# An MoE routing loop: the equality products go from VectorE to GpSimd, and the room left per expert from a running PSUM sum to a tile in SBUF

## What is computed

```python
logits = x @ w_gate                      # 1536 tokens, 8 experts
order = np.argsort(-logits.flatten())
for idx in order:
    tok, e = (int(idx) // E, int(idx) % E)
    if assigned[tok] >= 0 or counts[e] >= cap:     # cap = 192
        continue
    assigned[tok] = e
    counts[e] += 1
```

## Time and profile before

| | us |
|---|---|
| median of three runs | 922.08 |
| the three runs | 913.54, 922.09, 922.08 |
| time of the profiled execution | 913.54 |
| its span in the trace | 911.9 |
| outside the span (difference) | 1.6 |

### The profile page before, as it was taken

One profiled execution on the slowest core, in us unless ns is written; L12 is line 12 of the kernel. 1 busy time (PEld: TensorE's weight loads), 2 busy tenths in 40 slices (PEclk: granted clock), 3 DMA queues, 4 the chain that ended last, 5 costly groups with the idle time before them and its releaser, 6 DMA issues.

```text
span 911.9 us, 16773 instructions
## 1 busy us (share of the span) xinstructions
PE 751.2 (82%) x5353; PEld 661.4 (73%) x5354; DVE 381.5 (42%) x913; ACT 280.4 (31%) x536; POOL 99.1 (11%) x114
## 2 busy tenths in 40 slices
PE   3999996444444099999999667999999999999993
PEld 2898995334443099999999565887788788888882
DVE  5444443999988000000000382644444462536221
ACT  2455653000000022332222302443344452535210
POOL 2000000000000500000000001222122212122220
PEclk9999997555555589999999857999999999999997
DMA  9700002900000446666660301645264453454211
GB/s 219 206 2 1 1 2 70 407 35 0 0 0 0 163 138 212 230 228 224 244 231 27 110 0 36 214 128 149 57 202 136 138 160 93 127 138 120 53 27 30
DMA packets 63908, 103.91 MB, mean 114 GB/s; under 512 B 22336, under 2 KB 24384, under 8 KB 63872
## 3 DMA queue, kind: packets, MB, share of 16 engines
q1 hardware_dynamic: 54896, 80.05, 26.9%
q0 software_dynamic: 8976, 23.39, 10.0%
HBM read 87.64 MB, written 16.57 MB: 114 GB/s over the span
## 4 chain that ended last, share of the span: by engine, by line
PE 73%; issue 18%; DMA 3%; DVE 2%; POOL 1%; ACT 0%; SPq 0%; DVEq 0%; POOLq 0%; ACTq 0%
PE PS L737 12%; PE PS L739 11%; PE PS L738 11%; PE PS L670 9%; PE PS L659 8%; PE PS L502 4%; PE PS L465 3%; PE PS L482 3%; PE PS L733 3%; DMA XE<-routed_rows 2%; PE PS L717 2%; PE PS L726 1%; PE PS L443 1%; POOL routed_rows L391 1%; PE PS L680 1%
## 5 line engine op out<-in xcount | busy, mean ns | idle before, releaser
L1141 DVE TENSOR_TENSOR WS<-STAGE,WS 128x1024 f32 (+1 forms) x64 | 74.7, 1221 | 232.6 <-ACT WS L872 197.1
L737 PE MATMUL PS<-WS,XH 128*128 128x512 f32 x216 | 89.7, 415 | 3.9 <-DVE XL L1257 2.0
L620 PE MATMUL PS<-OH,arena 128*128 128x8 bf16 x1008 | 39.8, 169 | 61.2 <-DVE arena L1119 59.2
L659 PE MATMUL PS<-XTm,arena 128*128 128x192 f32 x512 | 88.4, 333 | 1.1 <-ACT XTm L855 1.1
L737 PE MATMUL PS<-WS,HH 128*128 128x512 f32 x216 | 88.8, 411 | 0.0
L659 PEld LDWEIGHTS PS<-XTm,arena 128*128 128x128 f32 x512 | 85.8, 195 | 1.3 <-issue 1.3
L739 PE MATMUL PS<-WS,XL 128*128 128x512 f32 x216 | 85.4, 395 | 0.0
L670 PE MATMUL PS<-HTm,arena 128*128 128x192 f32 x512 | 84.8, 327 | 0.5 <-ACT HTm L861 0.5
L738 PE MATMUL PS<-WS,XH 128*128 128x512 f32 x216 | 85.0, 394 | 0.0
L739 PE MATMUL PS<-WS,HL 128*128 128x512 f32 x216 | 84.6, 392 | 0.0
L738 PE MATMUL PS<-WS,HH 128*128 128x512 f32 x216 | 84.4, 391 | 0.0
(11 more groups left out here) (227 smaller groups left out, 1140.7 us busy)
## 6 DMA issues: line engine op xcount, KB each, us to landing
arena<-in_moe_w SPq DMA_DIRECT2D x16, 2048.0 KB, 8.9
STAGE<-in_moe_w SPq DMA_DIRECT2D x128, 256.0 KB, 4.8
XE<-routed_rows SPq DMA_DIRECT2D x8, 390.8 KB, 9.8
arena<-in_v SPq DMA_DIRECT2D x12, 256.0 KB, 6.4
out<-YO POOLq DMA_DIRECT2D x1, 3072.0 KB, 20.3
first_mixture<-YR POOLq DMA_DIRECT2D x16, 192.0 KB, 4.4
arena<-in_q SPq DMA_DIRECT2D x2, 1024.0 KB, 7.7
arena<-in_k SPq DMA_DIRECT2D x2, 1024.0 KB, 8.5
```

The costliest lines, as they stand in the source:

```text
L620: ins = pe.matmul(PS[:, 6, u * E:(u + 1) * E], CMP[:, t, u * P:(u + 1) * P], OH[:, t, :], start=False, stop=(t == NT - 1 and u == NT - 1), ...
L659: ins = pe.matmul(PS[:, 2 + f % 2, 0:CAP], W1[:, pp, c, f * P:(f + 1) * P], XTm[:, c, :], start=(c == 0), stop=(c == KD - 1))
L737: pe.matmul(acc, high, w_high, start=first, stop=False)
L1141: dve.tensor_tensor(part(1), STAGE[:, slot].rearrange("p o w f -> p (o w) f"), part(0).bitcast(F32), ALU.subtract)\
```

## The change

`TOTB` goes, `NEW` and `ROOM` come. `ROOM` holds for each expert the places that are left, begins at 192 and is kept in SBUF in fp32; PE no longer carries sums from one round to the next. The equality step leaves DVE: POOL gets a loop of its own over the 7 rounds, which waits for all three parts of `VROW`, makes `EQ` in 12 instructions of 128 columns, waits for them, and makes `EQD` in one of 1536. `PER` goes from 11 to 16.

```diff
         ASG = sb("ASG", [P, NT, E], BF16)
         UNA = sb("UNA", [P, NT])
-        TOTB = sb("TOTB", [P, E], BF16)
+        NEW = sb("NEW", [P, NT])
+        ROOM = sb("ROOM", [P, E])
         RED = sb("RED", [P, E])
         PEN = sb("PEN", [P, E])
...
                            YO[:, 0:1, :].broadcast_to([P, NT, DM])).then_inc(sm["yscat"], 16)
 
-            pool.memset(TOTB[:], 0.0).then_inc(sm["totb"], 1)
+            with pool.Fori(0, E - 1) as ph:
+                pool.wait_ge(sm["vrow"], ph * 3 + 3)
+                pool.sem_inc(sm["pool_held"], 1)
+                for t in range(NT):
+                    ins = pool.tensor_scalar(EQ[:, t * P:(t + 1) * P], VROW[:, t * P:(t + 1) * P], V[:, t:t + 1], None,
+                                             ALU.is_equal)
+                ins.then_inc(sm["pool_seq"], 1)
+                pool.wait_ge(sm["pool_seq"], ph + 1)
+                pool.tensor_tensor(EQD.rearrange("p (t n) -> p t n", t=NT), EQ.rearrange("p (t n) -> p t n", t=NT),
+                                   mid(upto[:], NT), ALU.mult).then_inc(sm["eqd"], 1)
 
             pool.wait_ge(sm["slot"], 1)
...
                               start=False, stop=False, skip_group_check=True)
 
-            pe.wait_ge(sm["totb"], 1)
-            pe.matmul(PS[:, 7, 0:E], ones_b[:], TOTB[:], start=True, stop=False, skip_group_check=True).then_inc(sm["tot"], 1)
             with pe.Fori(0, E - 1) as ph:
 
...
                                            V[:, 4 * c + i:4 * c + i + 1].broadcast_to([P, P]), ident[:])
                     ins.then_inc(sm["vr_done"], 1)
-                pe.wait_ge(sm["totb"], ph + 2)
-                pe.matmul(PS[:, 6, 0:NT * E], ones_b[:], mid(TOTB[:], NT), start=True, stop=False, skip_group_check=True)
                 for t in range(NT):
                     if t == NT - 1:
...
                     for u in range(NT):
                         ins = pe.matmul(PS[:, 6, u * E:(u + 1) * E], CMP[:, t, u * P:(u + 1) * P], OH[:, t, :],
-                                  start=False, stop=(t == NT - 1 and u == NT - 1), skip_group_check=True)
+                                  start=(t == 0 and u == 0), stop=(t == NT - 1 and u == NT - 1), skip_group_check=True)
                 ins.then_inc(sm["cnt"], 1)
                 pe.wait_ge(sm["noh"], ph + 1)
-                for t in range(NT):
-                    ins = pe.matmul(PS[:, 7, 0:E], ones_b[:], NOH[:, t, :], start=False, stop=(t == NT - 1), skip_group_check=True)
-                ins.then_inc(sm["tot"], 1)
+                pe.matmul(PS[:, 7, 0:NT * E], ones_b[:], NOH[:].rearrange("p t e -> p (t e)"), start=True, stop=True)\
+                    .then_inc(sm["tot"], 1)
 
             pe.wait_ge(sm["dstart"], 1)
...
             dve.wait_ge(sm["const"], NCONST)
             link(dve.memset(UNA[:], 1.0))
+            link(dve.memset(ROOM[:], float(CAP)))
             link(dve.memset(ASG[:], 0.0))
             link(dve.tensor_copy(LM[:], L0[:]))
             start = count[0]
-            PER = 11
+            PER = 16
             with dve.Fori(0, E - 1) as ph:
                 done = [0]
...
                 linked(dve.tensor_reduce(V[:], LM[:], AX.X, ALU.max))
                 dve.sem_inc(sm["best"], 1)
-                dve.wait_ge(sm["tot"], ph + 1)
-                dve.tensor_scalar(TOTB[:], bank(7, E), 1.0 / P, None, ALU.mult).then_inc(sm["totb"], 1)
                 linked(dve.tensor_tensor(EQW[:], LM[:], bc(V[:], E), ALU.is_equal))
                 linked(dve.tensor_tensor(EQW[:], EQW[:], mid(first[:], NT), ALU.mult))
...
                         greater(t)
                 dve.wait_ge(sm["vrow"], ph * 3 + 3)
-                dve.tensor_tensor(EQ.rearrange("p (t n) -> p t n", t=NT), VROW.rearrange("p (t n) -> p t n", t=NT), bc(V[:], P),
-                                  ALU.is_equal).then_inc(sm["eq"], 1)
-                dve.wait_ge(sm["eq"], ph + 1)
-                dve.tensor_tensor(EQD.rearrange("p (t n) -> p t n", t=NT), EQ.rearrange("p (t n) -> p t n", t=NT),
-                                  mid(upto[:], NT), ALU.mult).then_inc(sm["eqd"], 1)
                 for t in range(NT):
                     n = (t + 1) * P
...
                     ins.then_inc(sm["cmp"], 1)
                 dve.wait_ge(sm["cnt"], ph + 1)
-                linked(dve.tensor_reduce(VB[:], bank(6, NT * E).rearrange("p (t e) -> p t e", t=NT), AX.X, ALU.max))
-                dve.scalar_tensor_tensor(out=NOH[:], in0=bc(VB[:], E), scalar=CAP + 0.5, in1=OH[:], op0=ALU.is_lt, op1=ALU.mult)\
-                    .then_inc(sm["noh"], 1)
-                linked(dve.scalar_tensor_tensor(out=UNA[:], in0=VB[:], scalar=CAP + 0.5, in1=UNA[:], op0=ALU.is_gt, op1=ALU.mult))
-                dve.wait_ge(sm["noh"], ph + 1)
+                linked(dve.tensor_tensor(EQW[:], bank(6, NT * E).rearrange("p (t e) -> p t e", t=NT), mid(ROOM[:], NT),
+                                         ALU.is_gt))
+                linked(dve.tensor_reduce(VB[:], EQW[:], AX.X, ALU.max))
+                linked(dve.scalar_tensor_tensor(out=NEW[:], in0=VB[:], scalar=0.5, in1=UNA[:], op0=ALU.is_lt, op1=ALU.mult))
+                linked(dve.tensor_tensor(NOH[:], OH[:], bc(NEW[:], E), ALU.mult))
+                dve.sem_inc(sm["noh"], 1)
+                linked(dve.tensor_tensor(UNA[:], UNA[:], NEW[:], ALU.subtract))
                 linked(dve.tensor_tensor(ASG[:], ASG[:], NOH[:], ALU.add))
-                dve.wait_ge(sm["tot"], ph + 2)
-                linked(dve.tensor_scalar(PEN[:], bank(7, E), CAP - 0.5, -BIG, ALU.is_gt, ALU.mult))
+                dve.wait_ge(sm["tot"], ph + 1)
+                linked(dve.tensor_reduce(RED[:], bank(7, NT * E).rearrange("p (t e) -> p e t", t=NT), AX.X, ALU.add))
+                linked(dve.tensor_tensor(ROOM[:], ROOM[:], RED[:], ALU.subtract))
+                linked(dve.tensor_scalar(PEN[:], ROOM[:], 0.5, -BIG, ALU.is_lt, ALU.mult))
                 linked(dve.tensor_tensor(LM[:], L0[:], mid(PEN[:], NT), ALU.add))
                 assert done[0] == PER, done
             count[0] = start + PER * (E - 1)
 
-            link(dve.tensor_scalar(RED[:], bank(7, E), CAP - 0.5, None, ALU.is_lt))
+            link(dve.tensor_scalar(RED[:], ROOM[:], 0.5, None, ALU.is_gt))
             link(dve.tensor_tensor(EQW[:], mid(RED[:], NT), bc(UNA[:], E), ALU.mult))
             link(dve.tensor_tensor(ASG[:], ASG[:], EQW[:], ALU.add))
```

More of the change, by code:

```diff
@@ L203, in build @@
             dve noise_in tok_in zero_y xt_done xt_out lg_done lg_out
-            dstart best vr_done vrow cmp eqd cnt noh tot eq totb slot_ps slot scat xe0 xe1 w1a
+            dstart best vr_done vrow cmp eqd pool_seq cnt noh tot slot_ps slot scat xe0 xe1 w1a
             w1b w2a w2b nz_in xt1_done xt1_out h_ps h_out y_ps y_out l2_ps l2_out yr_ps yr_out x2a x2b expz lnu expd
```

## The result

| | before, us | after, us |
|---|---|---|
| median | 918.12 (4 runs) | 945.22 (4 runs) |
| single runs | 913.54, 922.09, 922.08, 914.15 | 940.62, 946.34, 944.1, 954.69 |
| profiled execution, and its span | 913.54, 911.9 | 944.42, 942.9 |

The changed kernel is slower: the ratio is 1.031, with a 95% interval of 1.021 to 1.041. The forecast was 948 us in a range of 915 to 976. Some executions of a kernel come out over 1% slower than others of the same code; medians here are of all runs, ratios of the faster state alone, so the two can differ a little.

What follows compares the result with a forecast made beforehand. DVE was taken to bound the seven routing rounds: -2.66 + 0.95 + 6.1 = +4.4 us each, +30.7 in all, -1.0 once, so +29.7: 943.2 or 951.8 by starting level. Forecast 948 us, range 915 to 976.

Steps and rivals of the forecast that it cites:

- The equality step leaves DVE, -2.66: In each routing round, DVE no longer makes EQ and EQD, which takes 2.66 us off the bound.
- TOTB counts nothing but once: Removing DVE's TOTB step gains nothing in a steady round; an earlier first-round transpose gives -1.0 us once.
- The tail, +0.95: DVE's steps ending a round, from VB to LM before, grow from 1.59 to 2.54 us, without a wait for PE.
- POOL's own price, 6.1: POOL's equality work per round: 3.0 us comparisons, 3.0 product, 0.1 wait; bounds 4.5 and 9.5 us.
- DVE and POOL take turns: During a round's comparisons the two engines alternate on SBUF, so DVE's row grows by POOL's whole time, 6.1 us.
- each delays DVE by its own length: POOL's 13 instructions fit among DVE's 23 comparisons, each lengthening DVE's row by its full duration.
- the one for a POOL that is shut out: Profile sign: DVE's comparisons keep their durations and PE waits for POOL's EQD behind the last comparison.
- The case that the prediction held likeliest: In the rounds, POOL and DVE alternate at about 6.1 us of POOL work; range 932 to 962 us, chance 0.55.
- its second rival: Engines alternate in the rounds, but POOL's work costs 9.5 us: +53.5 us, so 967 or 975.6; chance 0.12.
- its third: Only half of POOL's time in a round shuts DVE out: +8.4 us, so 922 or 930.5; chance 0.13.
- it doesn't matter for the sum who wins the turns: Whether POOL slips between DVE's comparisons or waits until they end, a round pays POOL's whole time; said to matter little.
- The memset at the kernel's start: DVE's memset beside POOL's iotas took 1.50 us, 0.44 more than a reading operation; weak evidence that DVE gives way.

Runs made afterwards that it cites:

- late run: The changed kernel, with POOL starting each round's equality work only after DVE has made all its comparisons; 983.23 us (one run).
- wide shadow: Against the shadow run: POOL's 12 unread comparisons became one subtraction of two tensors over 1536 columns, the product kept; 950.71 us, ratio 1.047.
- shadow run: Kernel before, DVE keeping all its work, while POOL also makes the 12 comparisons and the product on tiles nobody reads; 937.49 us, ratio 1.029.
- PSUM run: The changed kernel, with DVE's comparisons reading the transposes' PSUM banks instead of VROW in SBUF, POOL still reading VROW; 964.92 us (one run).

## Why the prediction was right

**What bounds the stage.** Right: the routing loses 34.2 us, and all other stages together lose nothing.

**The equality step leaves DVE, -2.66.** Right. In the late run, where POOL is quiet, the comparisons take 12.66 us in one piece without it, and 15.32 - 2.66 is just that.

**TOTB counts nothing but once.** Right. The first comparison starts 2.15 us after V in both kernels, and DVE now waits 0.32 us for ACT. Before, the first round is 1.17 us longer than the next (153.91 to 175.23, against 20.15); after, 25.22 against 25.18. So 1.13 us go once, where 1.0 was forecast.

**The tail, +0.95.** Right: 2.60 us in place of 1.59, and no wait for PE; the run with the tail alone gives +1.01.

**POOL's own price, 6.1.** Wrong in size. This is the term that was mis-sized: the twelve comparisons cost 7.0 us, not 3.0, because a POOL comparison with a per-partition value takes 0.58 us and not the 0.25 of the select. The product, guessed as 3.0, takes 3.08. P is 10.2 us, above the bound of 9.5. By the 4497 ns for 2048 columns in the Trainium skill (GPSIMD Engine Reference, § 3.1) the estimate had been 3.4 us, 10% too much here; that figure is for a sum in fp32, and the fp32 subtraction of the wide shadow took 3.02.

**DVE and POOL take turns.** Right that they contend, wrong in who pays. The step "each delays DVE by its own length" fails: nine POOL comparisons beside DVE stretch it by 1.0 us, about 0.1 us each of their 0.58. POOL pays by waiting, 1.17 us from one to the next over the twelve. Why a short POOL instruction costs DVE so much less than its length, and a long one nearly all that is left of it, no run here shows. Of the prediction's signs the one for a POOL that is shut out comes nearest: DVE's comparisons almost keep their durations, and PE waits for EQD behind the last of them, 5.85 us. The changed round in its parts, from the timeline:

| | us per round |
|---|---|
| equality step gone | -2.66 |
| comparisons stretched, 13.67 against 12.66 | +1.01 |
| from the last comparison (192.92) to EQD (198.28) | +5.36 |
| EQD to DVE's next step 0.90, where the last comparison to that step was 0.58 | +0.32 |
| tail | +1.01 |
| sum | +5.04 |
| measured (25.18 - 20.15) | +5.03 |

The last 0.32 is PE: it now has the 12 matmuls of `equals` and the last tile's 12 behind EQD, and had only the last tile's 12 behind the last comparison.

So POOL costs 6.7 us a round where the forecast had 6.1, and that the sum of 948 came so close to 945.22 is luck. Two errors met: POOL is dearer by 4.1 us, and 3.5 of its 10.2 us were hidden after all. The case that the prediction held likeliest, turns at a P of about 6.1, is not what happened; it is rather its second rival (a dearer POOL, there 9.5) and its third (only a part of POOL's time costs DVE's row, there half, here two thirds) at once, and either alone would have missed the time, at 967 or 922. The 7.5 that gives the likeliest case its upper end of 962 had no row behind it either. The prediction had said that it doesn't matter for the sum who wins the turns; that is wrong by 3.5 us a round. Held back until DVE has ended, as in the late run, POOL costs its whole 10.2 and the round is 29.2.

**The memset at the kernel's start**, on which the turns were forecast, pointed the right way, but it is still only one pair, and of instructions that only write. It may not be the same thing: in the shadow run a POOL memset of 1536 columns (164.40 to 165.81) lies beside DVE operations of 96 columns with two inputs, and they take 0.25 and 0.26 us as ever. What shows contention are the shadow runs, LM's 2.97 us above all, and the PSUM run, which turns it off.

## What to carry to other kernels

Work given to POOL beside DVE is not free because POOL is idle. Look at which DVE instructions will run beside it. Here one with two tensor inputs in SBUF (LM, 0.26 us, then 2.97) and comparisons at double pace with one input (0.68 us, then 3.18) were held until a long POOL instruction had ended. Short POOL instructions waited for DVE instead (0.58 us, then 1.17), and their result came late. With DVE reading PSUM neither held the other (POOL's twelve in 6.98 us). ScalarE met no such limit: its two passes for EQ took 5.1 us, POOL's twelve comparisons alone 7.0, and DVE's rows beside ScalarE stayed as they were. When the price of an operation is not in the trace, another operation of the same size is a poor stand-in; here the select (0.25 us) was off by a factor of 2.3 for the comparison (0.58).

## What the runs showed besides

The spread between runs of one kernel, some 10 us, was not understood at the prediction. In these ten profiles, each of another kernel but all alike up to the first V, it comes from the attention stage: the first V starts between 150.9 and 163.7 us, while the time from SLOT's end to the end of the span is 610 to 614 us in all of them. One stretch of the kernel before (its length, PE's busy time and instructions, granted clock, DMA share, GB/s), and the queries-times-keys matmul in the same stretch (busy us, mean ns):

```profile
40.00:50.00 10.00, 10.00 (x91) 1.00 0.02 3
...
L465 PE MATMUL PS<-arena 64*128 64x256 f32 x16 | 2.8, 428 | 0.0
```

and the same in the shadow run's profile, an execution of 946.81 us:

```profile
40.00:50.00 10.00, 10.00 (x50) 1.00 0.04 2
...
L482 PE MATMUL PS<-arena 64*128 64x256 f32 x8 | 2.4, 708 | 0.0
```

PE is busy all of the 10 us in both, and the granted clock is given as 1.00 in both, but the one makes 91 matmuls and the other 50, and the same form takes 428 and 708 ns. PE begins slow in every profile and becomes fast at a different moment, between 31 and 35 us in the first and between 51 and 55 in the second. The first V follows that moment: in the profiles where this form is slow last at 24.5 to 27.7 us it starts at 150.9 to 152.1, in the first one (31.3) at 153.9, and in the two where it is slow until 51 us, the shadow run and the late one, at 163.2 and 163.7. The granted clock's column doesn't show it; the durations do. What sets the moment was not tried. It is also why the rounds, which repeat within 0.05 us, are a better measure here than the total.
